# Row 5's end transposes ahead of T51, and th4, Cp5, Cd5 ahead of C51, in a hand-ordered attention and adapter kernel

## The chip, the cores and the metric

One core of one Trainium2 chip runs the kernel. The metric is the device time of one execution in microseconds (us), as the median of several runs. Beside it there is one profiled execution, whose trace gives every instruction's start and duration.

## What is computed

Two stages follow each other over a batch of 8 "rows" (batch entries). The first is windowed attention with 8 heads of 576 tokens and 64 features; four heads see the last 32 tokens, the other four every fourth of the last 128. The second is a mixture of eight rank-16 adapters of which each token takes its two best, added to the attention output.

```python
scores = scale * np.matmul(q, k.transpose(0, 1, 3, 2))
scores = np.where(masks[None, :, :, :], scores, -1000000000.0)
attn = np.exp(scores - max);  attn /= sum;  x = attn @ v      # 8 x 576 tokens, 512 wide
logits = x @ w_gate
topk = np.argpartition(-logits, K, axis=1)[:, :K]             # K = 2 of 8
w = softmax over the two;  delta[mask] += w * ((x @ A[e]) @ B[e])
return x + delta
```

## The kernel before

The work is cut into some 400 named operations. `Program.add` records each with its engine, the operations that it depends on and the PSUM bank that it uses; `PLAN`, a text written by hand, gives one order for all of them. Each engine takes its own operations in the order of that text, and `Program.run` puts a semaphore wait before an operation whose inputs come from another engine. The number behind `@` in the text is the first of the eight PSUM banks that the operation takes. Whoever takes a bank waits for all users of the operation that had it before (`ordered` adds these dependences through `held`). So the text sets both the order on each engine and the waits for banks.

For row r and head group g (0 or 1) the operations are, with their engine and the line that the profile shows:

- `Lq`, `Lv` (POOL, L296): DMA loads of q/k and of v. For row 7 these are four loads of q/k and four of v.
- `S0rg`, `S1rg` (PE, L236, `ps<-in` with a mask product `ps<-con,one` or `ps<-one` ahead): scores of the first five and the last four segments. `E0rg`, `E1rg` (ACT, L374): their exponentials, 960 and 768 elements wide.
- `Vrg` (PE, L236, `ps<-in,p`, 26 products, three banks): attention times v. `Rrg` (DVE, L410) takes the reciprocal of the sums, `Nrg` (DVE, L413) scales the result from PSUM into `x`, and `Brg` (POOL, L420) makes a bf16 copy `xb`.
- `Tr0`, `Tr1` (PE, L437, 8 transposes each) and `Ur` (PE, L461, 2 transposes for the 64 tokens at the end): they turn `xb`. `Cr0` (ACT, L447), `Cr1` (ACT, L450), and for the end tokens `Cdr` (ACT, L467) and `Cpr` (ACT, L471), copy the result from PSUM into `xt`.
- `Z0r`, `Z1r` (PE, L236, `ps<-aw,xt`, 12 and 8 products): adapter and gate products, in one bank each; `Y0r`, `Y1r` (ACT, L495) copy them to `zs`.
- `m0r`, `m1r`, `s12r`, `topr`, `ttr` (DVE, L507 to L515) find the two best gates; `thr` (ACT, L514) is a tanh of `tt`; `g2r` (DVE, L517) makes the gate weights from `th` and `top`, printed as `g<-th,top`. `gzr` (POOL, L522) weighs the adapter products; `Gr` (PE, L527) transposes them, `gnr` and `gcr` (ACT, L546, L543) copy them.
- `Dr0` to `Dr2` (PE, `ps<-bt,gn` or `ps<-bt,gc`): the second adapter product; `Ar0` to `Ar3` (DVE L574, POOL L602 and L582) add it to `x`; `dxr`, `dyr` (ACT, L600, L580) copy it out of PSUM where POOL does the addition. `Or` (SP) stores a row.

Rows overlap: while row 7's attention runs, row 6's values and row 5's adapter stage stand between its operations. The change lies there. Three places of the text bear on it. `V60@0`, `T51@3`, `V61@4`, `U5@7` are the PE operations just ahead of `S171@2`, the first scores of row 7. `V61@4` holds banks 4, 5 and 6 until `N61` has read them, and the next users of these banks are `Z15@6` and `S071@4`. `S171@2` takes banks 2 and 3, of which bank 3 was that of `T51`, so it also waits for `C51`. `U5@7` takes the bank that `T50` and `C50` had, and `Z05@7` takes it next.

The waits come about like this:

```python
if o.bank is not None and o.bank.users[0] == name:
    o.bank.at = int(at)
    for b in range(o.bank.at, o.bank.at + o.bank.size):
        o.deps = o.deps + held[b]
        held[b] = list(o.bank.users)
...
for s, v in waits.items():
    engines[o.eng].wait_ge(s, v)
```

Of the kernel before, what the change touches and what calls it, by code (L numbers as in the profile page):

```python
# [645 lines left out]
N51 R50 D22@5 N50 U4@7 gz3 Cd4 Cp4 G3@6 gn3 D21@3 gc3 A22 A21  # L646
Z04@7 Y04 B50 Lq711 S060@0 D32@2 Z14@7 S161@5 m04 E060 Y14 m14 E161 s124
S160@0 A32 Lv710 T50@7 E160 D30@3 S061@5 top4 V60@0 A30 tt4 R60 C50 Lv711
O1 E061 B51 T51@3 N60 C51 V61@4 th4 g24 R61 N61 U5@7 S171@2 Cp5
Cd5 S070@0 Z05@7 E171 E070 Z15@6 Y05 S170@2 S071@4 Y15 Lv700 m05 m15 top5  # L650
Lv701 B60 gz4 E170 E071 s125 G4@0 B61 D31@6 tt5 th5 gn4 V70@1 T60@4
A31 gc4 V71@5 U6@0 C60 O0 g25 O2 gz5 G5@4 Cp6 Cd6 R70 N70
B70 T61@2 D41@0 D42@3 R71 N71 gn5 A41 C61 dx4 gc5 B71 Bx7 D40@5
# [73 lines left out]
```

How the kernel before makes its waits and increments, by code:

```python
    def run(self, nc, text):  # L124
# [28 lines left out]
            mine = know[o.eng]  # L153
            waits = {s: v for s, v in need.items() if mine.get(s, 0) < v}
            for name in o.deps:
                d = self.ops[name]
                if d.sem in waits and waits[d.sem] >= d.count:
                    for s, v in d.know.items():
                        if s in waits and s != d.sem and waits[s] <= v:
                            del waits[s]
            for s, v in waits.items():
                engines[o.eng].wait_ge(s, v)
            for name in o.deps:
                d = self.ops[name]
                if d.eng == o.eng == "PE":
                    continue
                for s, v in d.know.items():
                    mine[s] = max(mine.get(s, 0), v)
                mine[d.sem] = max(mine.get(d.sem, 0), d.count)
            done = o.emit()
            if o.work[0] == "dma":
                sem = nc.alloc_semaphore(f"dma_{len(dmas)}")
                for i in done:
                    i.then_inc(sem, 16)
                o.sem, o.count = sem, 16 * len(done)
                dmas.append((sem, o.count))
            else:
                for i in done:
                    i.then_inc(sems[o.eng], 1)
                count[o.eng] += len(done)
                o.sem, o.count = sems[o.eng], count[o.eng]
            o.know = dict(mine)
        for s, v in dmas:
            if know["POOL"].get(s, 0) < v:
                nc.gpsimd.wait_ge(s, v)
```

## Time and profile before

| what | value |
|---|---|
| time, median of 3 runs | 99.39 us (99.38 to 100.11) |
| the profiled execution's own time | 100.05 us |
| its span, first to last instruction | 98.3 us |
| busy: PE, ACT, DVE, POOL | 82%, 73%, 65%, 56% of the span |
| mean granted TensorE clock | 0.977 of full speed |

Busy shares are averages over the span and name no bound by themselves. The timeline of one engine gives start, duration, engine, line and names of its instructions in order of time; what stands in brackets is the idle time before a row and the engine that ended it. The start of a DVE or ACT row can lie up to 0.1 us before the end of the row ahead of it on the same engine. The chain of waits goes back from the last instruction, at each step to what released it.

### The profile page before, as it was taken

The page shows a single profiled execution, that of the slowest core. Times are in us where ns is not written, and L with a number is a line of the kernel's source. Part 1 is how long each engine was busy: PE and PEld are TensorE (multiplying, and loading weights), DVE is VectorE, ACT ScalarE, POOL GpSimd, SP SyncE. Part 2 cuts the span into 40 slices and gives each one's busy share as a digit, 9 for nine tenths or more (in the row PEclk, how much of TensorE's full clock was granted, in tenths as well). Part 3 has the DMA queues.
Part 4 walks back from the last instruction along what each step waited for, and adds up shares of the span by engine and source line. Part 5 has one row for each costly group of instructions (what it writes and reads, how often), then busy time and mean ns, then how long its engine had stood idle before and what let it go on. Part 6 is the DMA issues. An engine that isn't in the chain of part 4 may idle for free.

```text
span 98.3 us, 3633 instructions
## 1 busy us (share of the span) xinstructions
PE 80.7 (82%) x1587; PEld 59.5 (61%) x1587; DVE 63.4 (65%) x138; ACT 71.4 (73%) x123; POOL 54.6 (56%) x73
## 2 busy tenths in 40 slices
PE   3999968868578989989998989999969989776500
PEld 2443646456455766679776859878757878564300
DVE  5770008606467269448766678789994999979810
ACT  5294791399938992896799598999769989957300
POOL 5999903670459317501945198099184464665820
PEclk9999999999999999999999999999999999999955
DMA  2999999999999999999999999999979999997894
GB/s 38 303 197 198 197 216 209 226 203 216 215 211 214 213 212 216 212 215 216 218 212 214 214 219 211 215 207 205 204 225 416 416 412 420 408 375 287 362 410 194
DMA packets 6095, 24.50 MB, mean 249 GB/s; under 512 B 832, under 2 KB 960, under 8 KB 5440
## 3 DMA queue, kind: packets, MB, share of 16 engines
q0 software_dynamic: 3920, 14.23, 72.7%
q1 hardware_dynamic: 2016, 9.77, 24.4%
q10 hardware_dynamic: 144, 0.28, 0.9%
q8 instruction: 12, 0.20, 0.7%
q14 instruction: 3, 0.02, 0.1%
HBM read 29.07 MB, written 9.44 MB: 392 GB/s over the span
## 4 chain that ended last, share of the span: by engine, by line
PE 30%; DMA 22%; ACT 17%; POOL 11%; DVE 11%; issue 3%; POOLq 0%
PE ps L236 26%; DMA in<-in_qkv_dram 22%; ACT p L374 9%; POOL in L296 7%; DVE x L413 4%; DVE x L574 4%; PE ps L437 3%; POOL xb L420 2%; ACT xt L447 2%; ACT gn L546 2%; POOL x L582 1%; ACT zs L495 1%; ACT gc L543 1%; PE ps L527 1%; DVE rec L410 1%
## 5 line engine op out<-in xcount | busy, mean ns | idle before, releaser
L420 POOL CAST xb<-x 128x1152 bf16<-128x1152 f32 (+1 forms) x16 | 18.3, 1143 | 24.3 <-DVE x L413 24.3
L374 ACT ACTIVATE p<-ps 128x960 bf16<-128x960 f32 (+1 forms) x32 | 27.5, 896 | 3.6 <-PE ps L236 3.3
L236 PE MATMUL ps<-in,p 128*64 128x130 bf16 (+1 forms) x416 | 21.4, 221 | 4.4 <-ACT p L374 3.8
L413 DVE TENSOR_TENSOR x<-ps,rec 128x1152 f32<-128x1152 f32 x16 | 21.7, 1358 | 0.6
L236 PEld LDWEIGHTS ps<-in,p 128*64 128x64 bf16 (+1 forms) x416 | 17.1, 104 | 7.9 <-ACT p L374 5.0
L574 DVE TENSOR_TENSOR x<-x,ps 128x1024 f32<-128x1024 f32 (+1 forms) x16 | 17.5, 1116 | 3.5 <-PE ps L236 3.5
L410 DVE RECIPROCAL rec<-ps 128x18 f32<-128x18 f32 x16 | 4.3, 270 | 16.1 <-PE ps L236 15.9
L522 POOL TENSOR_TENSOR gz<-zs,g 128x640 bf16<-128x640 f32 x7 | 8.9, 1274 | 10.3 <-DVE g L517 10.1
L236 PE MATMUL ps<-warm 128*128 128x512 f32 x22 | 12.2, 693 | 1.5 <-DVE warm L240 1.5
L296 POOL DMA_DIRECT2D in<-in_qkv_dram x22 | 11.8, 581 | 0.8 <-POOLq L710 0.8
L236 PEld LDWEIGHTS ps<-in 64*64 64x64 bf16 x576 | 10.7, 106 | 2.0
L236 PE MATMUL ps<-in 64*64 64x96 bf16 (+1 forms) x576 | 11.5, 200 | 0.0
L236 PE MATMUL ps<-aw,xt 128*128 128x136 bf16 x160 | 11.3, 223 | 0.2
L447 ACT COPY xt<-ps 128x1024 bf16<-128x1024 bf16 x8 | 8.1, 1010 | 4.0 <-PE ps L437 3.9
L236 PEld LDWEIGHTS ps<-aw,xt 128*128 128x128 bf16 x160 | 9.6, 98 | 1.0 <-ACT xt L447 0.4
L437 PE MATMUL ps<-one,xb 128*128 128x128 bf16 x128 | 9.5, 219 | 0.1
L437 PEld LDWEIGHTS ps<-one,xb 128*128 128x128 bf16 x128 | 7.6, 97 | 1.4 <-issue 0.5
L236 PEld LDWEIGHTS ps<-warm 128*128 128x128 f32 x22 | 4.5, 221 | 6.0 <-issue 4.5
L236 PE MATMUL ps<-bt,gn 128*128 128x256 bf16 (+1 forms) x48 | 6.8, 263 | 1.5 <-ACT gn L546 0.8
L236 PE MATMUL ps<-bt,gc 128*128 128x256 bf16 (+1 forms) x48 | 6.6, 255 | 1.5 <-ACT gc L543 1.5
L450 ACT COPY xt<-ps 128x1024 bf16<-128x1024 bf16 x7 | 7.2, 1035 | 0.5 <-PE ps L437 0.5
L495 ACT COPY zs<-ps 128x408 f32<-128x408 f32 (+1 forms) x14 | 5.9, 459 | 2.2 <-PE ps L236 2.2
(55 smaller groups left out, 102.7 us busy)
## 6 DMA issues: line engine op xcount, KB each, us to landing
in<-in_qkv_dram POOLq DMA_DIRECT2D x5, 1152.0 KB, 22.8
out_dram<-x SPq DMA_DIRECT2D x5, 1152.0 KB, 8.4
in<-in_qkv_dram POOLq DMA_DIRECT2D x10, 292.5 KB, 23.6
in<-in_qkv_dram POOLq DMA_DIRECT2D x10, 288.0 KB, 8.9
out_dram<-x SPq DMA_DIRECT2D x5, 576.0 KB, 3.0
in<-in_qkv_dram POOLq DMA_DIRECT2D x10, 146.2 KB, 8.2
in<-in_qkv_dram POOLq DMA_DIRECT2D x2, 434.2 KB, 14.5
out_dram<-x SPq DMA_DIRECT2D x1, 320.0 KB, 3.4
```

Source lines behind the costliest of these rows:

```text
L236: return nc.tensor.matmul(o, lhsT=lhsT, rhs=rhs, start=start, stop=stop, skip_group_check=True)
L296: nc.gpsimd.dma_start(out=IN[r % SLOTS][half(a), at : at + n], in_=qkv[r, a, :, at - 2 * VB * a : at - 2 * VB * a + n],)
L374: return [nc.scalar.activation(p[:, :, :].rearrange("p h (s c) -> p h s c", c=PER)[:, :, b0 : b0 + nb, 0:SEG], PS[:, k.at : k.at + 2, 0 : ...
L410: rc = add(f"R{tag}", "DVE", ("el", 60), lambda: [nc.vector.reciprocal(rec[:, :].rearrange("p (b i) -> p b i", b=3), PS[:, k.at : k.at + 3 ...
L413: nm = add(f"N{tag}", "DVE", ("el", XG), lambda: [nc.vector.tensor_tensor(X[r][:, XG * g : XG * g + XG].rearrange("p (b i n) -> p b i n", ...
L420: add(f"B{tag}", "POOL", ("el", cut), lambda: [nc.gpsimd.tensor_copy(XB[r % 2][:, g, 0:cut], X[r][:, XG * g : XG * g + cut])], [nm] + free)
L437: nc.tensor.transpose(tp[j][:, 128 * u : 128 * u + 128], xb[:, g, 256 * u + 128 * j : 256 * u + 128 * j + 128], ident())
L447: return [nc.scalar.copy(xt[:, 0:2, 0:S].rearrange("p j (c i) -> p j c i", c=C)[:, :, :, 0:128], tp.rearrange("p j (i c) -> p j c i", c=C))]
L450: return [nc.scalar.copy(xt[:, 2:4, 0:512], tp)]
L495: zc.append(add(f"Y{st}{r}", "ACT", ("el", len(us) * ZW), lambda us=us, k=k: [nc.scalar.copy(zs[:, us[0] : us[-1] + 1].rearrange("p u n -> ...
L522: return [en.tensor_tensor(GZ[i][:, us[0] : us[0] + n, :].rearrange("p u (e r) -> p u e r", e=E), zv()[:, us[0] : us[0] + n, 0:ER].rearran ...
L574: return [nc.vector.tensor_tensor(v, v, PS[:, k.at : k.at + nk].rearrange("p b n -> p (b n)"), ALU.add)]
```

## The change

Only the order text `PLAN` is edited: `U5@7` goes ahead of `T51@3`, and `th4`, `Cp5`, `Cd5` go ahead of `C51`. No operation is added or removed, and every bank stays the same.

```diff
-O1 E061 B51 T51@3 N60 C51 V61@4 th4 g24 R61 N61 U5@7 S171@2 Cp5
-Cd5 S070@0 Z05@7 E171 E070 Z15@6 Y05 S170@2 S071@4 Y15 Lv700 m05 m15 top5
+O1 E061 B51 U5@7 th4 Cp5 Cd5 T51@3 N60 C51 V61@4 g24 R61 N61 S171@2
+S070@0 Z05@7 E171 E070 Z15@6 Y05 S170@2 S071@4 Y15 Lv700 m05 m15 top5
```

On PE, between the values of row 6 and the scores of row 7, the order changes as follows. The first two rows are `V60`; the removed rows are `T51` (L437), `V61` (18 and 8 products) and `U5` (L461); the branch stands just ahead of `S171`.

```order
 L236 MATMUL ps<-in,p 64x130 x18
 L236 MATMUL ps<-in,p 128x130 x8
-L437 MATMUL ps<-one,xb 128x128 x8
-L236 MATMUL ps<-in,p 64x130 x18
-L236 MATMUL ps<-in,p 128x130 x8
-L461 MATMUL ps<-one,xb 128x128 x2
+L461 MATMUL ps<-one,xb 128x128 x2
+L437 MATMUL ps<-one,xb 128x128 x8
+L236 MATMUL ps<-in,p 64x130 x18
+L236 MATMUL ps<-in,p 128x130 x8
 L136 UNCONDITIONAL_BRANCH
```

The two products of `U5` have gone from behind `V61` to ahead of `T51`.

On ACT, the first row is `C50` and the second `E061`; L450 is `C51`, L514 `th4`, L471 and L467 the two copies of `U5`'s result; the two rows at the end are `E171` and `E070`.

```order
 L447 COPY xt<-ps 128x2x4x128
 L374 ACTIVATE p<-ps 128x2x5x96
-L450 COPY xt<-ps 128x2x512
 L514 ACTIVATE th<-tt 128x40
 L471 COPY xt<-ps 128x2x64
 L467 COPY xt<-ps 128x2x4x16
+L450 COPY xt<-ps 128x2x512
 L374 ACTIVATE p<-ps 128x2x4x96
 L374 ACTIVATE p<-ps 128x2x5x96
```

`C51` has gone behind the tanh and the two small copies. The orders on DVE, POOL and SP are the same in both kernels.

## Rows read from the trace of the kernel before

**Rows 1.** Chain of waits, 60 to 84 us: start us, us, what.
```profile
65.12 6.79 DMA in<-in_qkv_dram
...
72.00 1.75 PE ps L236 x52
73.75 0.02 issue
73.76 1.51 PE ps L236 x52
...
77.81 1.29 PE ps L236 x26
...
83.72 0.67 DVE top L515
```

**Rows 2.** Timeline of PE: start us, us, instruction, count, [idle before, releaser].
```profile
67.84 1.33 PE L236 MATMUL ps<-in,p 128*64 128x130 bf16 x26
69.23 0.61 PE L437 MATMUL ps<-one,xb 128*128 128x128 bf16 x8
69.77 1.34 PE L236 MATMUL ps<-in,p 128*64 128x130 bf16 x26
70.95 0.27 PE L461 MATMUL ps<-one,xb 128*128 128x128 bf16 x2
72.00 0.36 PE L236 MATMUL ps<-con,one 64*64 64x384 bf16 x4 [0.77 <-DMA in<-in_qkv_dram]
...
76.03 1.33 PE L236 MATMUL ps<-in,p 128*64 128x130 bf16 x26
```

**Rows 3.** Timeline of PE's weight loads around Z15.
```profile
73.23 0.34 PEld L236 LDWEIGHTS ps<-aw,xt 128*128 128x128 bf16 x5
73.76 0.47 PEld L236 LDWEIGHTS ps<-aw,xt 128*128 128x128 bf16 x8 [0.20 <-DVE x L413]
```

**Rows 4.** Timeline of DVE, 69 to 78 us.
```profile
69.01 0.19 DVE L512 SCALAR_TENSOR_TENSOR tt<-zs,s 128x40 f32<-128x40 f32 x1
...
69.51 1.36 DVE L413 TENSOR_TENSOR x<-ps,rec 128x1152 f32<-128x1152 f32 x1
71.06 1.08 DVE L517 SCALAR_TENSOR_TENSOR g<-th,top 128x40 f32<-128x40 f32 x1 [0.19 <-ACT th L514]
72.06 0.26 DVE L410 RECIPROCAL rec<-ps 128x18 f32<-128x18 f32 x1
72.35 1.36 DVE L413 TENSOR_TENSOR x<-ps,rec 128x1152 f32<-128x1152 f32 x1
...
77.27 0.19 DVE L517 SCALAR_TENSOR_TENSOR g<-th,top 128x40 f32<-128x40 f32 x1
```

**Rows 5.** Timeline of POOL, 66 to 84 us.
```profile
66.70 1.19 POOL L420 CAST xb<-x 128x1152 bf16<-128x1152 f32 x1
...
70.94 1.15 POOL L420 CAST xb<-x 128x1152 bf16<-128x1152 f32 x1 [2.08 <-DVE x L413]
72.22 1.27 POOL L522 TENSOR_TENSOR gz<-zs,g 128x640 bf16<-128x640 f32 x1
73.77 1.14 POOL L420 CAST xb<-x 128x1152 bf16<-128x1152 f32 x1 [0.28 <-DVE x L413]
...
83.61 0.73 POOL L602 TENSOR_TENSOR x<-x,awf 128x256 f32<-128x256 f32 x1 [1.40 <-ACT awf L600]
```

**Rows 6.** Timeline of ACT, 67 to 73 us.
```profile
67.51 1.02 ACT L447 COPY xt<-ps 128x1024 bf16<-128x1024 bf16 x1
68.40 1.00 ACT L374 ACTIVATE p<-ps 128x960 bf16<-128x960 f32 x1
69.88 1.01 ACT L450 COPY xt<-ps 128x1024 bf16<-128x1024 bf16 x1 [0.47 <-PE ps L437]
70.79 0.24 ACT L514 ACTIVATE th<-tt 128x40 f32<-128x40 f32 x1
71.26 0.27 ACT L471 COPY xt<-ps 128x128 bf16<-128x128 bf16 x1 [0.24 <-PE ps L461]
71.42 0.27 ACT L467 COPY xt<-ps 128x128 bf16<-128x128 bf16 x1
```

**Rows 7.** Timeline of ACT by shape, 74.9 to 75.6 us.
```profile
74.99 0.81 ACT L374 ACTIVATE p<-ps 128x768 bf16<-128x768 f32 x1
```

## The prediction

> **What bounds the kernel now.** I read the page first (PE is busy 82% of the span, which names no bound by itself), then the chain of waits, and then the timelines of the four engines from 67 to 78 us, because the edit moves instructions there alone. In the chain [rows 1] the reader is to see a DMA: the last q/k load of row 7 is issued at 65.12 and released S171 at 72.00, and from there PE carries the chain until V71 ends at 79.10 (77.81 + 1.29). PE's timeline says the same from its side [rows 2]: behind U5 it sits idle for 0.77 us until the DMA lands. So all that PE, ACT and DVE do between 69.2 and 71.7 has slack towards that landing, and moving work about within this slack gains nothing through S171.
>
> Behind 72.00 the chain has one small break: 73.75, "issue" 0.02, then PE again [rows 1]. The weight loads show what it is [rows 3]. The first load of Z15 starts at 73.76, 0.20 us after the last one of Z05, and was released by DVE's L413, which is N61 (72.35 + 1.36 = 73.71 [rows 4]): Z15 takes bank 6, which was V61's. Products of this kind follow each other by some 0.06 us (8 loads in 0.47 [rows 3]), so Z15 starts 0.18 us late. That is the only wait behind the landing that the edit can reach.
>
> Why is N61 so late? V61 was done at 71.11 [rows 2], but R61 starts at 72.06 [rows 4]. Between them stands g24, which took 1.08 us on a 40-wide tile, where g25, the same instruction of the next row, took 0.19 [rows 4]. g24 began at 71.06, released by th4, and ended at 72.14; POOL's cast B60 ran from 70.94 to 72.09 [rows 5]. So g24, which reads two tiles of SBUF, began just behind B60 and did not end before it.
>
> The Trainium skill, page "SBUF — State Buffer", section "Who interferes with whom", states this as a rule: a VectorE instruction with two SBUF inputs and a GpSimd instruction that reads SBUF exclude each other, and whichever is issued first keeps the shared ports until it ends. The 1.08 us agrees with it; by that rule g24 would take its short time if it began ahead of B60, and no row of this trace shows that order.
>
> **The change part by part.** *U5 ahead of T51.* V60 ends at 69.17, C50, from which U5 needs the bank, at 68.53 [rows 6], and B51, its input, at 67.89 [rows 5]; U5 waits for nothing. Its two products take 0.11 to 0.14 us of issue (by the 0.06 of rows 3 each, or by T51, whose eight start at 69.23 with V61 behind them at 69.77, 0.07 each); I take 0.11, so T51 goes to 69.34 and V61 to 69.88, ending at 71.21 instead of 71.11. PE's order ends at the same time and its idle time stays 0.77 us: nothing gained and nothing lost there.
>
> *th4, Cp5, Cd5 ahead of C51.* E061 ends at 69.40 and ACT then idled 0.47 us [rows 6]. tt4 is ready at 69.20 [rows 4], so th4 runs from about 69.35 to 69.55 in that hole, the two copies of U5 (0.27 each, overlapping by 0.1) until about 69.95, and C51, whose T51 ends at 69.95 (69.34 + 0.61), from 69.97 to 70.98. Before, C51 ended at 70.89: 0.09 later is what the move costs C51. S171 needs it for bank 3, and does not start before 72.00: 1.0 us of cover. If that cover were gone, the cost would be those 0.09 us. Z05 needs all four copies; they were done by 71.69 and now are by 70.98, neither late for its start after 72.8.
>
> *What th4's move does on DVE.* g24 is behind N60, which ends at 70.87 [rows 4]. Before, th4 came 0.19 us after that, and then B60 had begun. Now th4 is done over a us earlier, and g24 can follow N60 at once, at 70.79 to 70.98 with the usual overlap and the 0.19 us of g25. B60 has to be released by the same N60 and began 0.07 us after its end (70.94). The bounds of g24 are then 0.19 us, if its head start is enough, and about 1.3 us (70.79 to 72.09), if B60 is first all the same. I take 0.19: an order of events with a head start of 0.07 us, on an instruction of which all but 0.04 us is over when B60 starts. R61 then waits for V61 only: 71.24 to 71.50, N61 71.54 to 72.90. That is 0.81 us earlier than before.
>
> *What is late next.* With N61 out of the way, Z15 follows Z05 at 73.58. Of 0.81 us only 0.18 us counts, because the landing at 72.00 sets Z05. Next, does the rest follow? V70 stands at 76.03 [rows 2] and would go to 75.85; it needs E170, which ended at 75.80 [rows 7] and is held by ACT's own order, not by PE: just enough, and a first place where some hundredths could be lost. From V70 on, PE, DVE and ACT follow each other (V71 ends at 79.10, R71 follows), so the 0.18 us should reach the end. POOL's gz4 can start at the end of B60, 72.09 instead of 72.22, and B61 starts at gz4's end, about 73.4 instead of 73.77; neither is waited for soon. The loads on POOL's queue were issued by 69 us and are untouched.
>
> *Sum.* U5: 0. C51: 0 (0.09 under a cover of 1.0). Z15's wait: -0.18, with bounds 0 and -0.18 at this landing time. The profiled execution took 100.05 us, of which 98.3 are span and 1.75 lie around it; it would take 99.87. It stands 0.66 above the median of the runs, 99.39; the same 0.18 off the median gives 99.2.
>
> **The rivals.** *The change does nothing: g24 is held all the same.* If B60's claim is first although it starts later, g24 ends near 72.1 as before, N61 stays at 73.71, and the time is 99.39. For it speaks that 0.07 us of head start is little and that no row shows the order; against it that a DVE instruction already running has never been seen longer than 0.2 us with POOL idle at its start (g25).
>
> *The gain is larger, because the landing moves.* Z15 in the kernel before could not start ahead of N61's end, whatever the DMA does. If in unprofiled runs the load lands earlier by x, S171, S070 and Z05 move up by x (PE is free from 71.22, so x up to 0.77), the kernel before still stops at 73.76, and the changed one goes to 73.58 - x, until N61 (72.90) holds it at 72.95. The gain is then up to 0.81, and the time 98.6. If the load lands later by 0.18 or more, the gain is nothing. For an early landing speaks only that the other runs are shorter than the profiled one; against it, that an earlier landing does not shorten the kernel before by more than the few hundredths around Z15.
>
> *Slower: top6 loses against a POOL addition.* Late in the chain top6 takes 0.67 us on it [rows 1] and begins at 83.72, 0.11 us after POOL's A52 began at 83.61 [rows 5], and ends with it; next to the undisturbed 0.19 of an instruction of the same width [rows 4] this costs about 0.5 us. Here it has lost already; but if in the median runs top6 is ahead of A52 (they are 0.66 us shorter), the edit could turn the order, since A52 hangs on ACT and top6 on DVE: once ACT's chain gains the 0.18 us and DVE's less, A52 comes first. It decides at a difference of 0.0 between the two starts, and costs 0.5 - 0.18: 99.7 us. Against it: both chains hang on V71 and should move alike.
>
> **How the numbers follow.** The forecast of 99.2 gets a chance of 0.58, the rival without effect (99.39) 0.18, the larger gain (98.6 to 99.0) 0.12, the slower one (99.7) 0.12. The range has to hold the unknown landing on one side and top6 on the other; the runs before alone spread up to 100.11, so that a median at the upper level less 0.18 would be 99.9. I take 98.6 to 99.9. A change of under 1% (98.4 to 100.4) is about what a measurement of this kernel can't tell from none. No case worked out passes these ends; for cases not seen I leave 0.05 for faster and 0.04 for slower, and 0.91 for the same.
>
> **What would show it.** In the profile after: g24 at 70.8 with 0.2 us; R61 right behind V61; N61 ending near 72.9; no idle time ahead of Z15's first weight load; S171 still released by the DMA near 72.0; C51 ending near 71.0; V70 at 75.85. Wrong would be: g24 again over 1 us long; S171 released by ACT (C51); a wait on E170 ahead of V70 that gives the 0.18 back; or a time outside the range, which would mean that something the edit doesn't touch, such as the landing of the loads, moved with it.

## The result, and the profile after

The changed kernel takes 99.34 us in the median of 22 runs (98.67 to 100.12); the kernel before, in 22 runs beside them, 99.92 us (99.38 to 100.36). The ratio is 0.9947 with a 95% interval of 0.9928 to 0.9967: a gain of 0.5 us by this ratio (0.58 by the two medians), under 1%, with an interval that lies wholly below 1. The profiled execution took 98.79 us with a span of 97.0 us. Executions that lie over 1.5% above the fastest of their kernel are left out of the medians and ratios below.

The chain of waits of the changed kernel, at the places of [rows 1]:

```profile
66.63 2.24 PE ps L236 x54
68.87 0.11 PE ps L461 x2
68.98 0.48 PE ps L437 x8
69.47 1.27 PE ps L236 x26
70.74 0.03 issue
70.77 3.24 PE ps L236 x104
...
76.54 1.29 PE ps L236 x26
...
82.45 0.67 DVE top L515
```

The DMA row of [rows 1] is gone. S171 starts at 70.77 right behind V61, so in this execution the load had landed before PE came to it. Its chain from V60 to V71 is PE's alone, though the weight loads further down show a short wait that the chain doesn't. The timeline of PE, beside [rows 2]:

```profile
67.54 1.33 PE L236 MATMUL ps<-in,p 128*64 128x130 bf16 x26
68.71 0.27 PE L461 MATMUL ps<-one,xb 128*128 128x128 bf16 x2
68.85 0.62 PE L437 MATMUL ps<-one,xb 128*128 128x128 bf16 x8
69.40 1.34 PE L236 MATMUL ps<-in,p 128*64 128x130 bf16 x26
70.77 0.36 PE L236 MATMUL ps<-con,one 64*64 64x384 bf16 x4
...
74.76 1.33 PE L236 MATMUL ps<-in,p 128*64 128x130 bf16 x26
```

V60 starts 0.30 us earlier than before (67.54 for 67.84), ahead of anything that the edit moves, so this part of the difference between the two profiles is not the change's. From the start of V60 to the start of V71 it is 9.90 us before and 8.93 after: 0.97 of the 1.26 us between the two profiled executions lies there. The timeline of DVE, beside [rows 4]:

```profile
68.71 0.19 DVE L512 SCALAR_TENSOR_TENSOR tt<-zs,s 128x40 f32<-128x40 f32 x1
...
69.21 1.36 DVE L413 TENSOR_TENSOR x<-ps,rec 128x1152 f32<-128x1152 f32 x1
70.49 0.19 DVE L517 SCALAR_TENSOR_TENSOR g<-th,top 128x40 f32<-128x40 f32 x1
70.78 0.27 DVE L410 RECIPROCAL rec<-ps 128x18 f32<-128x18 f32 x1
71.08 1.36 DVE L413 TENSOR_TENSOR x<-ps,rec 128x1152 f32<-128x1152 f32 x1
```

g24 takes 0.19 us instead of 1.08, R61 starts as V61 ends (70.74), and N61 ends at 72.44. POOL, beside [rows 5], shows that B60 now begins after g24 and is not longer for it, and ACT, beside [rows 6], that th4 and U5's copies fill the idle time that stood in front of C51:

```profile
70.64 1.15 POOL L420 CAST xb<-x 128x1152 bf16<-128x1152 f32 x1 [2.08 <-DVE x L413]
71.75 1.28 POOL L522 TENSOR_TENSOR gz<-zs,g 128x640 bf16<-128x640 f32 x1
72.97 1.14 POOL L420 CAST xb<-x 128x1152 bf16<-128x1152 f32 x1
```

```profile
68.97 0.26 ACT L514 ACTIVATE th<-tt 128x40 f32<-128x40 f32 x1
69.10 0.29 ACT L471 COPY xt<-ps 128x128 bf16<-128x128 bf16 x1
69.24 0.31 ACT L467 COPY xt<-ps 128x128 bf16<-128x128 bf16 x1
69.50 1.01 ACT L450 COPY xt<-ps 128x1024 bf16<-128x1024 bf16 x1
```

The weight loads at Z15, beside [rows 3], are the row to stop at:

```profile
71.62 0.70 PEld L236 LDWEIGHTS ps<-aw,xt 128*128 128x128 bf16 x12
72.49 0.47 PEld L236 LDWEIGHTS ps<-aw,xt 128*128 128x128 bf16 x8 [0.16 <-DVE x L413]
```

Z15 is still held by N61, by 0.16 us, though N61 is early. Both sides of this wait have moved, N61 by the edit and Z05 by the landing. To take out the different starts, measure both from the start of B60, the cast that hangs on N60. Before, Z15 stood 73.76 - 70.94 = 2.82 us behind B60; now 72.49 - 70.64 = 1.85 us. N61 has been brought forward by 0.97 us, of which the landing of the profile before would have let through only some 0.2 us.

### The profile page after: what moved, and what is told of

Its sections match the earlier page's. It is cut to its first block, busy times and chain, and to the rows that moved or that the text cites. A ratio compares the mean times of both kernels' runs of the same rounds, so it can differ in the third digit from the quotient of the medians.

```text
span 97.0 us, 3633 instructions
## 1 busy us (share of the span) xinstructions
PE 81.2 (84%) x1587; PEld 59.7 (62%) x1587; DVE 62.4 (64%) x138; ACT 71.0 (73%) x123; POOL 54.5 (56%) x73
## 4 chain that ended last, share of the span: by engine, by line
PE 55%; ACT 25%; DVE 9%; POOL 3%; issue 2%; POOLq 0%
PE ps L236 48%; ACT p L374 14%; PE ps L437 5%; DVE x L574 4%; DVE x L413 3%; ACT zs L495 2%; ACT xt L447 2%; ACT gn L546 2%; PE ps L527 1%; POOL x L582 1%; ACT gc L543 1%; ACT in L286 1%; POOL xb L420 1%; PE ps L461 1%; ACT xt L450 1%
## 5 line engine op out<-in xcount | busy, mean ns | idle before, releaser
L236 PE MATMUL ps<-warm 128*128 128x512 f32 x22 | 12.9, 729 | 1.5 <-DVE warm L240 1.5
L437 PE MATMUL ps<-one,xb 128*128 128x128 bf16 x128 | 9.5, 219 | 0.1
L437 PEld LDWEIGHTS ps<-one,xb 128*128 128x128 bf16 x128 | 7.5, 98 | 1.4 <-POOL xb L420 0.7
L450 ACT COPY xt<-ps 128x1024 bf16<-128x1024 bf16 x7 | 7.2, 1035 | 0.0
```

What stands on the lines that cost most here:

```text
L236: return nc.tensor.matmul(o, lhsT=lhsT, rhs=rhs, start=start, stop=stop, skip_group_check=True)
L437: nc.tensor.transpose(tp[j][:, 128 * u : 128 * u + 128], xb[:, g, 256 * u + 128 * j : 256 * u + 128 * j + 128], ident())
L450: return [nc.scalar.copy(xt[:, 2:4, 0:512], tp)]
```

## The experiments

**Theory A** is the prediction's mechanism: g24 was held by B60, this held R61 and N61, and these held Z15; how much of it is gained depends on when the last q/k load lands. **Rival B**: the gain is that of U5 and its copies, out of the way of S171 and E171. **Rival C**: the landing differs from execution to execution, and the edit does nothing. A third rival, that the edit itself brings the landing forward, was not set against these; what the profiles say of it stands with the account of N61 and Z15 below.

**The parts.** th4 alone goes ahead of C51:

```diff
-O1 E061 B51 T51@3 N60 C51 V61@4 th4 g24 R61 N61 U5@7 S171@2 Cp5
+O1 E061 B51 th4 T51@3 N60 C51 V61@4 g24 R61 N61 U5@7 S171@2 Cp5
```

> One part alone: th4 goes ahead of C51; U5, Cp5 and Cd5 stay where they were. Theory A (th4 ready before N60 ends, so that g24 runs ahead of B60 and N61 ends some 0.8 us earlier): g24 0.2 us long just behind N60, Z15 no longer held 0.2 us or more by N61 at a like landing, and the whole gain of the change, a ratio of 0.993 to 0.997 to the kernel before. Rival B (the gain is from U5 and its two copies being out of the way of S171 and E171): g24 may be short, the ratio is 1.000. Rival C (the gain is a difference of landing times that has nothing to do with the edit): 1.000.

U5, Cp5 and Cd5 alone are moved:

```diff
-O1 E061 B51 T51@3 N60 C51 V61@4 th4 g24 R61 N61 U5@7 S171@2 Cp5
-Cd5 S070@0
+O1 E061 B51 U5@7 Cp5 Cd5 T51@3 N60 C51 V61@4 th4 g24 R61 N61 S171@2
+S070@0
```

> The other part alone: U5 ahead of T51, Cp5 and Cd5 ahead of C51, th4 behind C51 as before. Theory A: th4 ends near 71.0, g24 begins behind B60 and is 1.0 to 1.1 us long, N61 ends as in the kernel before, ratio 1.000 (within 0.002). Rival B: ratio 0.993 to 0.997. Rival C: 1.000.

Another cure for the same wait; th4 stays late, but g24 goes behind N61 on DVE:

```diff
-O1 E061 B51 T51@3 N60 C51 V61@4 th4 g24 R61 N61 U5@7 S171@2 Cp5
+O1 E061 B51 T51@3 N60 C51 V61@4 th4 R61 N61 g24 U5@7 S171@2 Cp5
```

> The kernel before with another cure of the same wait: g24 goes behind N61 on DVE, th4 and all else stay. Theory A (what matters is that R61 and N61 don't stand behind a g24 that is held by POOL): R61 starts right behind V61, N61 ends some 0.8 us earlier, ratio 0.993 to 0.997; gz4 starts about 0.8 us later and is not waited for. Rival B: 1.000. Rival C: 1.000.

And the whole change beside them:

> The change as a whole once more, on the same chip as its parts. Theories A and B: ratio 0.993 to 0.997. Rival C: 1.000 within 0.002.

Measured on one chip: before 99.79 us; th4 alone 99.37 (ratio 0.9971, 0.9938 to 1.0004); U5 alone 99.79 (1.0003, 0.9968 to 1.0038); g24 behind 99.48 (0.9976, 0.9946 to 1.0005); the whole change 99.31 (0.9976, 0.994 to 1.0012). The medians stand in the order that theory A has, but three ratios lie just above its 0.993 to 0.997, and every interval reaches 1, that of the whole change too: by their times alone these four runs decide nothing. Their profiles do decide who holds whom. DVE in the run with th4 alone, then with U5 alone, then with g24 behind N61:

```profile
70.14 0.19 DVE L517 SCALAR_TENSOR_TENSOR g<-th,top 128x40 f32<-128x40 f32 x1
70.51 0.27 DVE L410 RECIPROCAL rec<-ps 128x18 f32<-128x18 f32 x1 [0.17 <-PE ps L236]
```

```profile
71.20 1.15 DVE L517 SCALAR_TENSOR_TENSOR g<-th,top 128x40 f32<-128x40 f32 x1
72.28 0.26 DVE L410 RECIPROCAL rec<-ps 128x18 f32<-128x18 f32 x1
```

```profile
70.14 0.27 DVE L410 RECIPROCAL rec<-ps 128x18 f32<-128x18 f32 x1 [0.29 <-PE ps L236]
70.45 1.36 DVE L413 TENSOR_TENSOR x<-ps,rec 128x1152 f32<-128x1152 f32 x1
71.72 0.19 DVE L517 SCALAR_TENSOR_TENSOR g<-th,top 128x40 f32<-128x40 f32 x1
```

th4's place alone makes g24 short, and then R61 waits for PE instead of g24. Without it g24 is 1.15 us long, whatever U5 does. And g24 is short as well if it comes late enough for B60 to be over. Over all the profiles it is the same: where g24 starts 0.04 to 0.13 us behind B60 (five profiles), it takes 1.06 to 1.15 us and ends 0.04 to 0.05 us after B60; where it starts 0.15 us ahead of B60 (eight) or after B60's end (one), it takes 0.19. The step from there to Z15 can't be read here: in these three profiles the load landed 6.9 to 7.0 us after its issue, and Z15 follows Z05 without a wait in each, with U5 alone too. An early landing makes the step visible.

**The landing, early.** In the kernel before and in the changed one, the last q/k load brings a quarter of its columns:

```diff
-[load(f"Lq{r}{g}{h}", r, [(h, QK_AT[h][g], QK)], free) for h in range(2)]
+[load(f"Lq{r}{g}{h}", r, [(h, QK_AT[h][g], QK // 4 if g and h else QK)], free) for h in range(2)]
```

> The kernel before, but the last q/k load of row 7 brings a quarter of its columns, so that it lands about 1 us earlier; row 7's scores of one half of the heads then use old data. Theory A (Z15 starts at the later of the landing's chain and N61, and here N61 holds it): S171 starts about 1 us earlier relative to B50, the wait of Z15 for N61 grows from 0.2 to 0.8 to 1.0 us, and the time falls little, 99.4 to 99.6 (ratio 0.995 to 0.999). If the landing alone decided (C): 99.0, ratio 0.990.

> The changed kernel with the same short load (row 7's scores of one half of the heads use old data). Theory A: S171 follows V61 without a wait, Z15 is held by N61 0.2 us at most, time 98.6 to 98.9, which is 0.7 to 1.0 us under the kernel before with the short load. If the landing alone decided (C), both kernels with the short load have the same time.

The same load with one part of the change each:

> th4 alone ahead of C51, with the last q/k load of row 7 a quarter long (row 7's scores of one half of the heads use old data), where the whole change made 0.77 us. Theory A (th4 makes the gain): ratio 0.987 to 0.991 to the kernel before, as the changed kernel with the short load (0.9886); Z15 held by N61 0.3 us at most. Rival B (U5 and its copies): 0.998 as the kernel before with the short load, Z15 held about 1.0 us.

> U5, Cp5 and Cd5 alone moved, th4 behind C51, with the same short load (row 7's scores of one half of the heads use old data). Theory A: ratio 0.997 to 0.999, g24 over 1 us long, Z15 held by N61 about 1.0 us. Rival B: 0.987 to 0.991.

| last q/k load short | median, us (runs) | ratio to the kernel before (its load whole) |
|---|---|---|
| kernel before | 99.78 (12) | 0.9982 (0.9952 to 1.0012) |
| U5 alone | 99.71 (12) | 0.9996 (0.9965 to 1.0027) |
| th4 alone | 98.70 (7) | 0.9894 (0.9855 to 0.9933) |
| changed kernel | 99.01 (6) | 0.9886 (0.9841 to 0.9931) |

The first and last row were measured on one chip, beside a kernel before at 100.04 us, the two between on another, beside 99.65. The kernel before can't use an early landing: its time hardly falls. The changed kernel and th4 alone gain some 0.8 to 1.0 us, U5 alone nothing. Both times of the first pair are 0.1 to 0.2 us above what was expected, their difference is within it. The weight loads of Z15 and the start of B60 in the kernel before with the short load (one view each):

```profile
74.00 0.47 PEld L236 LDWEIGHTS ps<-aw,xt 128*128 128x128 bf16 x8 [1.02 <-DVE x L413]
```

```profile
71.18 1.15 POOL L420 CAST xb<-x 128x1152 bf16<-128x1152 f32 x1 [2.07 <-DVE x L413]
```

The wait that was 0.20 us has grown to 1.02, and Z15 stands 74.00 - 71.18 = 2.82 us behind B60, exactly where it stood with the whole load. That is N61's floor, and it doesn't move with the landing. In the changed kernel with the short load:

```profile
72.98 0.47 PEld L236 LDWEIGHTS ps<-aw,xt 128*128 128x128 bf16 x8 [0.16 <-DVE x L413]
```

```profile
71.12 1.15 POOL L420 CAST xb<-x 128x1152 bf16<-128x1152 f32 x1 [2.08 <-DVE x L413]
```

The floor there is 1.86 us behind B60. With U5 alone Z15 waits again. With th4 alone the view joins the twenty loads of Z05 and Z15 into one row, but they take 1.32 us and not the 1.18 that they take where nothing holds them (the late landing below); cut at 72.3 us, the view shows the eight of Z15 from 72.33 on, 0.15 us late and 1.93 us behind B60 (70.40):

```profile
73.55 0.47 PEld L236 LDWEIGHTS ps<-aw,xt 128*128 128x128 bf16 x8 [1.13 <-DVE x L413]
```

```profile
71.48 1.32 PEld L236 LDWEIGHTS ps<-aw,xt 128*128 128x128 bf16 x20
```

So th4 makes 0.89 of the 0.97 us at Z15, and U5 the other 0.08. Rival B is out: its part alone makes nothing where the whole makes 0.77 us (99.78 to 99.01). Rival C is out as well: two kernels with the same short load differ by it. The landing is not the gain, it decides how much of it is let through.

There is a second way to see this. In all the profiles V60 starts between 66.82 and 68.08 us, ahead of anything that the edit moves; this spread of 1.26 us is larger than the gain, and it is in every time above. From the start of V60 to that of V71 it is left out (one profiled execution each):

| kernel | last q/k load, issue to landing, us | V60 to V71, us |
|---|---|---|
| before | 6.8 | 9.90 |
| U5 alone | 7.0 | 9.95 |
| g24 behind N61 | 7.0 | 9.90 |
| th4 alone | 6.9 | 9.78 |
| whole change, two profiles | 5.7 and 5.3 | 8.93 and 8.94 |
| before, load short | 4.6 | 9.90 |
| U5 alone, load short | 4.8 | 9.90 |
| th4 alone, load short | 5.2 | 9.01 |
| whole change, load short | 5.1 | 8.94 |

From V71's start to the end of the span all of them take 20.5 to 20.7 us, so what is gained at V71 reaches the end.

**The landing, late.** The load goes behind two v loads on POOL's queue, in both kernels:

```diff
-Z04@7 Y04 B50 Lq711 S060@0 ... A32 Lv710 ... C50 Lv711
+Z04@7 Y04 B50 S060@0 ... A32 Lv710 ... C50 Lv711 Lq711
```

> The kernel before, but the last q/k load of row 7 is issued behind two v loads, so that it lands 0.7 to 1.4 us later. Theory A: S171 starts near 73, N61 is long done when Z15 comes, time 100.4 to 101.0 (ratio 1.004 to 1.012).

> The changed kernel with the same late load. Theory A: the same time as the kernel before with the late load, within 0.15 us, because the landing then sets both and N61 is waited for in neither. Rival B (a gain that does not hang on N61): 0.4 to 0.6 us under the kernel before with the late load.

Measured: 100.49 us for the kernel before (10 of 12 runs; ratio 1.0046, 1.0011 to 1.0082), 100.41 for the changed one (8 of 12; 1.0055, 1.002 to 1.0091). By the medians the changed kernel is 0.08 us faster, by the ratios 0.09 slower: both are within the 0.15 that was expected, and no gain is left that these runs can tell. PE and its weight loads in the kernel before, and then in the changed one:

```profile
72.99 0.36 PE L236 MATMUL ps<-con,one 64*64 64x384 bf16 x4 [1.58 <-DMA in<-in_qkv_dram]
```

```profile
73.85 1.18 PEld L236 LDWEIGHTS ps<-aw,xt 128*128 128x128 bf16 x20
```

```profile
72.48 0.36 PE L236 MATMUL ps<-con,one 64*64 64x384 bf16 x4 [1.91 <-DMA in<-in_qkv_dram]
```

```profile
73.34 1.18 PEld L236 LDWEIGHTS ps<-aw,xt 128*128 128x128 bf16 x20
```

In both, the DMA holds S171 by over 1.5 us, and the twenty loads run through: nothing waits for N61 any more, early or late.

**A step further.** The change makes Z05's inputs ready when V61 ends, so Z05 could fill the wait for the landing:

```diff
-S171@2 S070@0 Z05@7 E171 E070 Z15@6 Y05 S170@2
+Z05@7 Y05 S171@2 S070@0 E171 E070 Z15@6 S170@2
```

> The changed kernel, and Z05 with its copy Y05 ahead of S171 and E171: the change has made Z05's four inputs ready when V61 ends, so that Z05 (0.68 us) can fill the wait for the landing. Theory A with the landing as the next bound: S171 is released by the DMA or follows Z05, no wait for N61 is left ahead of Z15, V70 stands 0.3 to 0.5 us earlier behind the landing; time 98.8 to 99.1, ratio 0.988 to 0.993 to the kernel before. If PE's wait at the landing were covered anyway, the time is that of the changed kernel, ratio 0.995 to 0.998.

In addition, A52 goes behind gz6 on POOL:

```diff
-C71 T70@4 D51@5 A52 th6 g26 A51 D50@0 A50 C70 gz6 Z07@2
+C71 T70@4 D51@5 th6 g26 A51 D50@0 A50 C70 gz6 A52 Z07@2
```

> The same, and POOL's addition A52 goes behind gz6, so that top6 doesn't meet it. If a two-input DVE instruction is held by a POOL instruction that began before it, as g24 was by B60: top6 takes 0.2 instead of 0.75 us, th6 follows C71 without a wait (0.18 us before), time 0.1 to 0.2 us under the run with Z05 alone. If top6's length has another cause, it stays at 0.75 us.

Measured beside a kernel before at 99.65 us: 99.24 (ratio 0.9936, 0.9908 to 0.9963) with Z05 ahead, 99.15 (10 of 12 runs; 0.9939, 0.9907 to 0.997) with both. This beats the kernel before and the ratio lies between the two expectations; against the change itself (0.9947) it is no gain that these runs can tell. PE in the run with Z05 ahead, where the load landed 5.4 us after its issue, shows why it is no more there:

```profile
70.99 0.88 PE L236 MATMUL ps<-aw,xt 128*128 128x136 bf16 x12
71.80 0.36 PE L236 MATMUL ps<-con,one 64*64 64x384 bf16 x4
...
72.91 0.65 PE L236 MATMUL ps<-aw,xt 128*128 128x136 bf16 x8 [0.18 <-DVE x L413]
```

S171 follows Z05 without a wait, but Z15 then stands at N61's new floor again (72.91, with B60 at 71.06: 1.85 us): the wait for the landing that Z05 was to fill is not there. In the run with A52 moved as well the load landed late, after 6.8 us, and there the step pays: V71 starts 9.30 us behind V60, where th4 alone with a like landing took 9.78. With A52 moved, top6 fell from 0.75 us to

```profile
82.27 0.19 DVE L515 TENSOR_TENSOR top<-zs,mx 128x40 f32<-128x40 f32 x1
```

So top6 was held by a POOL instruction too. Of the gain the time shows nothing that these runs can tell. In the two profiles the way from V71's start to the start of POOL's last addition is 0.21 us shorter with A52 moved (14.78 us, 14.99 without), but from the end of that addition to the end of the span it is 5.05 us instead of 4.25, and output stores are what runs there. Whether moving A52 costs this or that execution alone had it, no run shows.

## Why the prediction was right, and where it was off

The direction, the range (98.6 to 99.9) and the class of under 1% held; the time forecast for the median, 99.2, was measured as 99.34.

*g24 by its order against B60.* Right: 0.19 us, as g25 in [rows 4]. The rule of the Trainium skill, page "SBUF — State Buffer", section "Who interferes with whom", that the instruction issued first keeps the ports, agrees with the trace after: g24 first, and short. (The two rows overlap by 0.04 us only, so this trace shows nothing of what POOL would have to wait.) The rival in which g24 is held all the same falls.

*U5 ahead of T51.* The sign was wrong. I charged 0.11 us to T51 and V61. Measured, V61 starts 1.86 us behind V60 (69.40 - 67.54), before 1.93 us (69.77 - 67.84 [rows 2]); with U5 alone it is 1.86 as well, with th4 alone 1.94. The step failed at "V60 ends at 69.17", as if T51 had followed V60 directly. DVE of the kernel before has the addition A30, from whose bank T51 takes over, and PE's weight loads the gap in front of T51:

```profile
67.88 1.21 DVE L574 TENSOR_TENSOR x<-x,ps 128x1024 f32<-128x1024 f32 x1
```

```profile
69.20 0.46 PEld L437 LDWEIGHTS ps<-one,xb 128*128 128x128 bf16 x8 [0.21 <-issue]
```

A30 ended at 69.09, and T51 came after it; the view itself names only "issue", the bank comes from the order text. U5 takes another bank and now runs in that gap: it is free there, and no longer stands behind V61. Why T51's weight loads then follow A30's end by 0.05 us and not by 0.11, which makes the 0.07 us, stays open.

*N61 and Z15.* N61's gain of 0.81 us was right but for U5: with the 0.18 us by which V61 came earlier than I had it, it makes 0.99, and 0.97 was measured at Z15's floor. The size of the result was off in the step that let only 0.18 us of it through, "because the landing at 72.00 sets Z05". That landing was the one execution's. From its issue, the load took 6.8 us there (65.12 to 71.9), 5.7 in the profile after (64.82 to 70.5), 5.3 in another profile of the changed kernel, and 7.0 in the one with U5 alone. With a landing early enough nearly the whole 0.97 us comes through, with a late one nothing. Two of the signs that were named for the profile after failed with this step: S171 was not released by the DMA near 72.0, and Z15's first weight load still had 0.16 us of idle time ahead of it. The median gain of 0.5 us lies between, so the forecast's 0.18 us was too small, and the prediction's second rival, the larger gain with an early landing, is a part of the answer and not a case of 0.12 beside it. My argument against it, that an early landing doesn't shorten the kernel before, was true and spoke for it: the kernel before was held at its floor, and the changed one is not.

What makes the landing differ from one execution to the next is left open; no run here varied it without touching the load. Nor is it shown that the edit has no part in it: with the load whole and in its place, the four profiles without the whole change have 6.8 to 7.0 us, and of the four with it (two of them with Z05 ahead as well) three have 5.3 to 5.7 and one 6.8. The load is issued at 65 us, ahead of what the edit moves, and lands behind it; eight executions are too few to tell. The short load shows the gain of N61 apart from this, but how much of the 0.5 us in the median it makes is not settled.

*C51 under the landing.* Right in kind: it ended at 70.51 and released nothing that was waiting, but its cover in this execution was 0.26 us to S171 at 70.77, not the 1.0 us that was worked out with the late landing.

*top6 as the slower rival.* It fell. top6 took 0.75 us or 0.76 in every profile with A52 in its old place, of the kernel before, the changed one and the experiments; it never came ahead of A52, so there was nothing to lose.

*From the profile to the median.* I took 0.18 us off a median of three runs, 99.39. Over 22 runs the median before was 99.92; the profiled execution, at 100.05, was no outlier. So the base was 0.53 us too low and the gain 0.40 us too small (0.18 for 0.58): that 99.2 came so near to 99.34 is two misses that cancel, and luck.

## What to carry to other kernels

A short instruction that takes five times its usual length is worth reading with the other engine's row beside it: here two tiles of SBUF were read on DVE while POOL worked, and a start some tenths of a us earlier, ahead of POOL's, was the cure. Where two waits end close together, like a landing and N61 here, the profile shows only the one that was later in that execution; work out the floor under it as well, since the other runs may stand on it. And where an effect drowns in the spread of the times, move the competing bound out of the way in both kernels: the short load raised what th4 alone gains from 0.3% to 1.1%. In the profiles, measure from a row just ahead of the edit, as from V60 here, so that what varies before it drops out.

## What was not expected of the hardware

The time from issue to landing of one and the same load differed by over a us between executions (5.3 to 7.0 us with an unchanged queue), though the kernels do not differ ahead of its issue. Whether what differs behind its issue plays a part is open. And B60 was not lengthened by starting close behind g24's start: 1.15 us in both profiles.
